# Layer 2's first projection by seven block products instead of eight

## The reference

```python
# attention: q, k, v [2, 8, 576, 64]; pooled (factor 4) plus a band of +-3 positions -> x [1152, 512]
h = x @ w_in                                  # layer 1: [1152, 512] @ [512, 2048]
g = np.where(h > 0.0, h, np.exp(np.minimum(h, 0.0)) - 1.0)
x = g @ w_out                                 # [2048, 512]
p = domain_probs / (domain_probs.sum(-1, keepdims=True) + 1e-09)
for e in range(4):                            # layer 2: 4 experts
    h = np.maximum(x @ w1[e], 0.0)            # [1152, 512] @ [512, 1024]: its first projection
    out += p[:, e:e + 1] * (h @ w2[e])        # [1024, 512]: the projection back
```

## Time and profile before

| | |
|---|---|
| median of 3 runs | 693.27 us (692.98 to 693.93) |
| span of the profiled execution | 692.0 us |
| TensorE busy | 678.2 us (98%) |
| VectorE, ScalarE, GpSimd busy | 300.9, 245.5, 217.4 us |
| layer 1, batch 1 (4 blocks) | from 189.83 to 292.55 us |
| layer 2 (8 halves) | from 292.55 us to the end |

### The profile page before, as it was taken

How to read it: one execution, slowest core, us unless ns; L and a number is a source line. 1 busy time by engine, 2 the same in 40 slices (tenths; PEclk the granted TensorE clock), 3 DMA queues, 4 the chain that set the end, 5 groups by cost and what they waited for, 6 DMA issues and landing times.

```text
span 692.0 us, 12297 instructions
## 1 busy us (share of the span) xinstructions
PE 678.2 (98%) x4558; PEld 625.7 (90%) x4564; DVE 300.9 (43%) x586; ACT 245.5 (35%) x665; POOL 217.4 (31%) x193
## 2 busy tenths in 40 slices
PE   7979999999999999999999999999999999999998
PEld 4659999999999999998898898998998998998986
DVE  3765666767695574542222222222222222223222
ACT  4664656556575474442031031130230220320310
POOL 5564444445437335222022022112211220220200
PEclk9998999999999999999999999999999999999999
DMA  9933161614212311311011011011011011000012
GB/s 207 191 79 96 62 143 54 166 38 143 62 62 62 118 65 61 122 62 62 0 62 62 0 61 61 0 61 61 0 61 61 0 61 61 26 35 0 0 43 93
DMA packets 51481, 46.01 MB, mean 66 GB/s; under 512 B 31616, under 2 KB 33920, under 8 KB 51456
## 3 DMA queue, kind: packets, MB, share of 16 engines
q1 hardware_dynamic: 51456, 45.67, 22.8%
HBM read 43.30 MB, written 2.36 MB: 66 GB/s over the span
## 4 chain that ended last, share of the span: by engine, by line
PE 89%; DVE 5%; ACT 2%; DMA 1%; issue 1%; POOL 1%; SPq 0%; DVEq 0%; ACTq 0%; POOLq 0%
PE psum L376 28%; PE psum L377 27%; PE psum L378 27%; PE psum L294 1%; DMA k_in<-in_k 1%; PE psum L368 1%; DVE h_lo L745 1%; PE psum L322 1%; ACT attn_p L527 1%; DVE elu_sum L739 1%; PE psum L281 1%; DVE x_lo L723 1%; DVE neg_max L688 1%; DVE elu_sum L733 1%; PE psum L313 1%
## 5 line engine op out<-in xcount | busy, mean ns | idle before, releaser
L376 PE MATMUL psum<-x_hi,wa_hi 128*128 128x384 f32 (+1 forms) x624 | 200.2, 321 | 0.0
L378 PE MATMUL psum<-x_hi,wa_lo 128*128 128x384 f32 (+1 forms) x624 | 199.2, 319 | 0.0
L377 PE MATMUL psum<-x_lo,wa_hi 128*128 128x384 f32 (+1 forms) x624 | 199.1, 319 | 0.0
L883 POOL TENSOR_TENSOR wb_lo<-wb_raw,wb_hi 128x512 fp32r<-128x512 f32 x64 | 85.4, 1339 | 239.7 <-ACT wb_hi L559 239.7
L599 ACT ACTIVATE h_hi<-psum 128x384 fp32r<-128x384 f32 x96 | 47.2, 492 | 291.3 <-PE psum L378 291.3
L376 PEld LDWEIGHTS psum<-x_hi,wa_hi 128*128 128x128 f32 x624 | 117.2, 188 | 0.9
L377 PEld LDWEIGHTS psum<-x_lo,wa_hi 128*128 128x128 f32 x624 | 117.2, 188 | 0.3
L378 PEld LDWEIGHTS psum<-x_hi,wa_lo 128*128 128x128 f32 x624 | 117.1, 188 | 0.0
L771 DVE SCALAR_TENSOR_TENSOR h_lo<-psum,h_hi 128x384 fp32r<-128x384 f32 x96 | 53.4, 558 | 143.7 <-ACT h_hi L599 143.7
L778 DVE SCALAR_TENSOR_TENSOR o_acc<-psum,gate_now,o_acc 128x512 f32<-128x512 f32 x72 | 54.1, 751 | 139.5 <-PE psum L378 139.5
L883 POOL TENSOR_TENSOR wa_lo<-wa_raw,wa_hi 128x512 fp32r<-128x512 f32 x60 | 76.0, 1300 | 121.5 <-ACT wa_hi L554 121.5
(11 more groups left out here) (94 smaller groups left out, 720.8 us busy)
## 6 DMA issues: line engine op xcount, KB each, us to landing
wa_raw<-in_moe_w_in SPq DMA_DIRECT2D x8, 1024.0 KB, 5.2
wb_raw<-in_moe_w_out SPq DMA_DIRECT2D x8, 1024.0 KB, 5.0
wa_raw<-in_moe_w SPq DMA_DIRECT2D x8, 1024.0 KB, 5.0
wb_raw<-in_moe_w SPq DMA_DIRECT2D x8, 1024.0 KB, 5.0
out<-o_acc SPq DMA_DIRECT2D x9, 256.0 KB, 2.0
q_in<-in_q SPq DMA_DIRECT2D x12, 144.0 KB, 4.0
k_in<-in_k SPq DMA_DIRECT2D x12, 144.0 KB, 4.1
v_in<-in_v SPq DMA_DIRECT2D x6, 288.0 KB
```

The source lines that it names most:

```text
L376: nc.tensor.matmul(bank_cols, w_hi(n), x_hi_(n), start=(n == 0), stop=False)
L377: nc.tensor.matmul(bank_cols, w_hi(n), x_lo_(n), start=False, stop=False)
L378: last = nc.tensor.matmul(bank_cols, w_lo(n), x_hi_(n), start=False, stop=(n == chunks - 1))
L883: nc.gpsimd.tensor_tensor(lo[:, c, :], raw[:, c, :], hi[:, c, :].bitcast(F32), ALU.subtract).then_inc(lo_ready, 1)
```

## The change

A half's first projection is done for each batch by itself (`step2`, two for a half). The operands are cut in 2 by 2 blocks: weights by 256 hidden columns and 256 channels, tokens by 288 tokens and 256 channels. In place of the 8 block products the result is put together from 7 (P1 to P7), with sums of weight blocks (S1, S2, S4 and, in place, one block of `wa_raw`), sums of token blocks (T1, T2, T4 and one block of `y_acc` in place) and sums of results. Each block product has two pairs p = 0, 1 (128 hidden columns each) of 6 matmuls with 288 columns.

The sums of weights (`add_w2`) are 4 GpSimd instructions for each half, queued behind the `wb` split, and there are 3 more operands to split (`s_hi`, `s_lo`). The sums of tokens (`add_y`) are 4 VectorE instructions for each batch, once, with 7 parts to split instead of 4, whose lo parts are moved to GpSimd (`split_y`). For batch 0 these stand inside block 4 of layer 1, before 4 blocks of work; for batch 1 they stand behind the last group of layer 1. The results' sums are VectorE instructions with one PSUM and one SBUF input; ScalarE copies P1 to SBUF. Three of the four hidden blocks then have their ReLU and lo part taken from SBUF sums. The projection back has 2 banks instead of 3. The buffers of the attention are given back to make room. `split_first2` puts the first split of layer 2's weights in groups 8 to 14 of block 7.

```diff
-DOWN2_BANKS = (0, 1, 2)
+DOWN2_BANKS = (7, 6)
+BANK_A, BANK_B, BANK_C = (0, 3), (1, 4), (2, 5)
...
-        elu_exp, elu_sum = sb("elu_exp", [128, 2, N1]), sb("elu_sum", [128, 2, N1])
+        sums2 = sb("sums2", [128, 3, PAIRS2, N2])
+        p1_sum, u2_sum, w_sum = sums2[:, 0], sums2[:, 1], sums2[:, 2]
...
+        s_raw = y_acc[:, 0:3, 0:2 * QF].rearrange("p s (k n) -> p s k n", k=2)
+
+        def t_raw(b, t):
+
+            return h_spare[:, T_RAW[t], b * SEQ:(b + 1) * SEQ].rearrange("p (k n) -> p k n", k=2)
...
+        def y_quad(b, kh, th):
+            return y_acc[:, 2 * kh:2 * kh + 2, b * SEQ + N2 * th:b * SEQ + N2 * (th + 1)]
...
+        def wa_quad(fh, kh):
+            return wa_raw[:, 2 * kh:2 * kh + 2, QF * fh:QF * (fh + 1)]
...
+            def step2(j, b):
+
+                v = 2 * j + b
...
+                pe.wait_ge(y_lo_ready, Y_PARTS * b + 2)
+                for p in range(PAIRS2):
+                    pe.wait_ge(h_lo_ready, UPS_LAYER1 + TILES_STEP * (v - 1) + p + 1)
+                    product2(bank(BANK_A, p), weights(0, 0, p), tokens(0, 0), True, False, p1_done)
+                pe.wait_ge(y_lo_ready, Y_PARTS * b + 3)
+                for p in range(PAIRS2):
+                    pe.wait_ge(moe_free, MOE_CREDIT + GROUPS_LAYER1)
+                    pe.wait_ge(c21_ready, PAIRS2 * v + p + 1)
+                    product2(bank(BANK_B, p), weight_sum(S2, p), token_sum(T2_), True, False, p6_done)
+                pe.wait_ge(y_lo_ready, Y_PARTS * b + 6)
+                for p in range(PAIRS2):
+                    pe.wait_ge(p1_copied, PAIRS2 * v + p + 1)
+                    product2(bank(BANK_A, p), weights(0, 1, p), tokens(1, 0), False, True, p2_done)
+                for p in range(PAIRS2):
+                    pe.wait_ge(c12_ready, PAIRS2 * v + p + 1)
+                    product2(bank(BANK_C, p), weight_sum(S1, p), token_sum(T1_), True, False, p5_done)
+                for p in range(PAIRS2):
+                    pe.wait_ge(u2_ready, PAIRS2 * v + p + 1)
+                    product2(bank(BANK_B, p), weights(1, 0, p), tokens(0, 1), False, False, p7_done)
+                for p in range(PAIRS2):
+                    pe.wait_ge(w_ready, PAIRS2 * v + p + 1)
+                    product2(bank(BANK_C, p), weight_sum(S4, p), tokens(1, 1), False, True, p3_done)
+                pe.wait_ge(y_lo_ready, Y_PARTS * b + 7)
+                for p in range(PAIRS2):
+                    pe.wait_ge(c22_ready, PAIRS2 * v + p + 1)
+                    product2(bank(BANK_B, p), weights(1, 1, p), token_sum(T4_), False, True, p4_done)
+
             def block2(e, half):
 
                 j = 2 * e + half
...
                 pe.wait_ge(wa_lo_ready, KC * (w + 1))
-                for g in range(UP2):
...
+            def split_first2(n):
+
+                act.wait_ge(wa_loaded, 16 * (2 * BLOCKS1 + 1))
+                act.wait_ge(group_done, groups_before1(2 * BLOCKS1 - 1) + UP1)
+                split_w2(0, n)
...
+                if n < KC:
+                    act.wait_ge(s_raw_ready, 4 * j + 3)
+                    nc.scalar.copy(wa_hi[:, n, :], wa_raw[:, n, :]).then_inc(wa_hi_ready, 1)
+                else:
+                    act.wait_ge(s_raw_ready, 4 * j + 4)
+                    nc.scalar.copy(s_hi[:, n - KC], s_raw[:, n - KC]).then_inc(s_hi_ready, 1)
...
+            def step2(j, b):
+
+                v = 2 * j + b
+                w = 2 * BLOCKS1 + j
...
+                def hidden_hi(fh, th, p, src):
+                    nc.scalar.activation(h_hi[:, 2 * fh + p, b * SEQ + N2 * th:b * SEQ + N2 * (th + 1)], src,
+                                         ACT.Relu).then_inc(h_hi_ready, 1)
+
+                for p in range(PAIRS2):
+                    act.wait_ge(p1_done, PAIRS2 * v + p + 1)
+                    act.wait_ge(h_lo_ready, UPS_LAYER1 + TILES_STEP * (v - 1) + 3 * PAIRS2 + p + 1)
+                    nc.scalar.copy(p1_sum[:, p], psum[:, BANK_A[p], 0:N2]).then_inc(p1_copied, 1)
+                if b == 0:
+                    split_wb(w, 0)
+                    split_wb(w, 1)
+                for p in range(PAIRS2):
+                    act.wait_ge(p2_done, PAIRS2 * v + p + 1)
+                    hidden_hi(0, 0, p, psum[:, BANK_A[p], 0:N2])
+                if b == 0:
+                    split_wb(w, 2)
+                for p in range(PAIRS2):
+                    act.wait_ge(c22_ready, PAIRS2 * v + p + 1)
+                    hidden_hi(1, 1, p, w_sum[:, p])
+                if b == 0:
+                    split_wb(w, 3)
+                for p in range(PAIRS2):
+                    act.wait_ge(c12_ready, UNIT_CREDIT + PAIRS2 * v + p + 1)
+                    hidden_hi(0, 1, p, u2_sum[:, p])
+                for p in range(PAIRS2):
+                    act.wait_ge(c21_ready, UNIT_CREDIT + PAIRS2 * v + p + 1)
+                    hidden_hi(1, 0, p, p1_sum[:, p])
...
                 if not last:
-                    for c in range(KC):
-                        split_wa(w + 1, c, GROUPS_LAYER1 + UP2 * (j + 1))
+                    act.wait_ge(wa_loaded, 16 * (2 * BLOCKS1 + j + 2))
+                    for n in range(KC + 3):
+                        split_w2(j + 1, n)
...
+                if n in (0, 1, 4, 5):
+                    c = n if n < 2 else n - 2
+                    act.wait_ge(t_raw_ready, 4 * b + 2)
+                    nc.scalar.copy(x_hi[:, c, b * SEQ:(b + 1) * SEQ],
+                                   y_acc[:, c, b * SEQ:(b + 1) * SEQ]).then_inc(y_hi_ready, 1)
+                else:
+                    t = {2: T2_, 3: T1_, 6: T4_}[n]
+                    act.wait_ge(t_raw_ready, 4 * b + {2: 3, 3: 1, 6: 4}[n])
+                    nc.scalar.copy(t_hi[:, t, :, b * N2:(b + 1) * N2], t_raw(b, t)).then_inc(y_hi_ready, 1)
...
-            act.wait_ge(moe_free, MOE_CREDIT + groups_before1(BLOCKS1))
-            for n in range(KC):
-                split_y(0, n)
+            after = {9 + n: [(split_y, 0, n)] for n in range(Y_PARTS)}
+            for g in range(GROUPS1):
+                group1(BLOCKS1, 1, g, after.get(g, ()))
+            with act.Fori(BLOCKS1 + 1, 2 * BLOCKS1 - 1) as w:
+                    group1(w, 1, g)
+            after = {UP1 + n: [(split_first2, n)] for n in range(KC + 3)}
+            for g in range(GROUPS1):
+                group1(2 * BLOCKS1 - 1, 1, g, after.get(g, ()), False)
+            for n in range(Y_PARTS):
                 split_y(1, n)
...
+                def add_p1(p, done, bank, dst, ready):
+                    dve.wait_ge(done, PAIRS2 * v + p + 1)
+                    dve.wait_ge(p1_copied, PAIRS2 * v + p + 1)
+                    nc.vector.tensor_tensor(dst[:, p], psum[:, bank[p], 0:N2], p1_sum[:, p], ALU.add).then_inc(ready, 1)
+
+                def hidden_lo(n, fh, th, p, src):
+                    at = (slice(None), 2 * fh + p, slice(b * SEQ + N2 * th, b * SEQ + N2 * (th + 1)))
+                    dve.wait_ge(h_hi_ready, UPS_LAYER1 + TILES_STEP * v + PAIRS2 * n + p + 1)
+                    nc.vector.scalar_tensor_tensor(h_lo[at], src, 0.0, h_hi[at].bitcast(F32),
+                                                   ALU.max, ALU.subtract).then_inc(h_lo_ready, 1)
+
+                for p in range(PAIRS2):
+                    add_p1(p, p6_done, BANK_B, u2_sum, u2_ready)
+                for p in range(PAIRS2):
+                    hidden_lo(0, 0, 0, p, psum[:, BANK_A[p], 0:N2])
+                for p in range(PAIRS2):
+                    add_p1(p, p5_done, BANK_C, w_sum, w_ready)
+                for p in range(PAIRS2):
+                    dve.wait_ge(p7_done, PAIRS2 * v + p + 1)
+                    dve.wait_ge(w_ready, PAIRS2 * v + p + 1)
+                    nc.vector.tensor_tensor(w_sum[:, p], psum[:, BANK_B[p], 0:N2], w_sum[:, p], ALU.add
+                                            ).then_inc(c22_ready, 1)
+                for p in range(PAIRS2):
+                    dve.wait_ge(p3_done, PAIRS2 * v + p + 1)
+                    dve.wait_ge(u2_ready, PAIRS2 * v + p + 1)
+                    nc.vector.tensor_tensor(u2_sum[:, p], psum[:, BANK_C[p], 0:N2], u2_sum[:, p], ALU.add
+                                            ).then_inc(c12_ready, 1)
+                    dve.wait_ge(y_lo_ready, Y_PARTS * (b + 1))
+                    hidden_lo(1, 1, 1, p, w_sum[:, p])
+                for p in range(PAIRS2):
+                    dve.wait_ge(w_ready, PAIRS2 * v + p + 1)
+                    add_p1(p, p4_done, BANK_B, p1_sum, c21_ready)
+                    hidden_lo(2, 0, 1, p, u2_sum[:, p])
+                for p in range(PAIRS2):
+                    hidden_lo(3, 1, 0, p, p1_sum[:, p])
+
...
+            def add_y(b, n):
+
+                if n == 0:
+                    dve.wait_ge(moe_free, MOE_CREDIT + groups_before1(BLOCKS1 * (b + 1)))
+                    nc.vector.tensor_tensor(t_raw(b, T1_), y_quad(b, 0, 1), y_quad(b, 0, 0), ALU.subtract
+                                            ).then_inc(t_raw_ready, 1)
+                elif n == 1:
```

(61 more changed lines are left out.)

145 lines of the change are left out of this document (90 added, 55 removed).

## The result

The changed kernel takes 713.34 us (median of 4 runs, 709.83 to 714.15); the kernel before, run beside it, 693.60 (692.98 to 695.10). The ratio is 1.028, 95% interval 1.025 to 1.031: slower by 20 us, twice the 10 of the forecast. It lies inside the stated range of 684 to 717, and just outside the 697 to 712 that the forecast gave itself. The profiled execution took 713.66 us, its span is 711.6.

What follows compares the result with a forecast made beforehand. TensorE, busy 98% of the span, was taken as the bound. The span, 692.0 - 20.7 - 0.3 + 18.2 + 3.9 + 3.6 + 2.5 + 3.2 = 702.4, plus 1.3 gave 703.7, forecast 703.5 us; range 684 to 717, its own 697 to 712.

Steps and rivals of the forecast that it cites:

- (b): Layer 1, blocks 4 and 5: late casts and GpSimd splits make TensorE wait for `wb_lo`, 3.6 us; bounds 2.5 and 5.3.
- The turns: Layer 2 halves: VectorE's two-SBUF-input instructions alternate with GpSimd's sums, 1.47 us a turn; stall 2.6 us in seven halves, 18.2 us.
- the timetable: Step-by-step times forecast for a half and the end of layer 1; in a half, lo parts end from 11.31 to 17.19 us.
- rival of cheap turns: VectorE instructions slip in beside GpSimd's without waiting out the hold; 679.4 us, or 685.5 if only halves are spared; chance 0.20.
- (a): Start of layer 2: ScalarE's seven batch 1 casts, queued before its first P1 copy, stall TensorE's P2 by 3.9 us.
- (c): Layer 1, block 7: the first half's `add_w2` falls among VectorE's pairs, stalling TensorE about 2.5 us; 2.0 to 3.6.
- (d): Around the end of layer 1: clock falls after the stalls of (a) and (b), 1.6 us each, 3.2 us; bounds 0 and 6.
- the clock falls in every half: Rival: the stall in each of 7 halves lowers the clock, 1.6 us each, 11 more: 715 us; chance 0.13.

Runs made afterwards that it cites:

- e1: Changed kernel with GpSimd's sums of weights held back until the half's last lo part is done; 686.6 us, ratio 0.989 to the kernel before.
- e8: Changed kernel with only the second two of the four weight sums of halves 2 to 8 held back; 698.07 us, ratio 1.007 to the kernel before.
- e2: Changed kernel with the weight sums of halves 2 to 8 replaced by one tiny sum and three write-only memsets; 685.65 us, ratio 0.987.
- e4: Changed kernel with batch 0's token casts behind block 4's weight casts and their lo parts behind the weight splits of blocks 5 and 6; 702.91 us.
- e7: e5 with the first half's weight sums also held back until block 7's last lo part, and TensorE's waits for split sums moved to P6 and P3; 680.49 us.
- e3: Changed kernel with batch 1's seven token casts moved on ScalarE from before the first P1 copy into the first half's first step; 708.8 us.
- e5: Changed kernel with the edits of e1, e3 and e4 together; 679.70 us, ratio 0.981 to the kernel before.

## Why the prediction was right, and short by ten

**The matmuls.** A first projection came down by 24.99 - 22.23 = 2.76 us, forecast 2.59: its 168 matmuls cost 132.3 ns each, not 133.3. The projection back stayed, at 24.50.

**The sum.** By span, 702.4 us was forecast and 711.6 measured. Of the 9.2 between them, 5.9 are the clock's falls from 190 us on, 3.2 the attention part and 1.1 the waits of layer 1; the matmuls gave 1.6 more than forecast, and 0.6 are left over. Two slips in the working change little: in (b), 41.5 - 38.4 is 3.1 and not 3.3, and the bounds of the terms add up to 696 and 713, not 697 and 712.

**The turns.** Right in mechanism and size: 2.6 us a half were forecast and 2.61 measured, with the lo parts' ends within 0.12 us of the timetable. Held back (e1), halved (e8) or made write-only (e2), the sums give back all, two thirds or all of it. The rival of cheap turns is out: L925 from SBUF took 766 ns on the mean beside the sums and 509 without. Two small errors cancel: GpSimd's sums took 1.37 to 1.50 us, longer than the 1.26 taken from the earlier trace rows, but a turn stayed at 1.46. In e1, away from such VectorE instructions, the sums took 1.28 to 1.30, so the rest is probably GpSimd's own wait for VectorE.

**The end of layer 1.** (a) 3.9 us forecast, 3.5 shown and 3.6 from start to start (310.81 - 303.99 less the 3.2 of P1 and P6). (b) 3.6 forecast, 3.45 shown, plus 0.72 for `wa_lo` of block 5, which the timetable had ready at 25.0 for a need at 25.6. (c) 2.5 forecast, 1.77 + 0.27 shown. The releasers are not the ones named: at block 5 the last was `h_lo` (VectorE, 236.04 us) where `wb_lo` was forecast (GpSimd's split ended at 235.7), and at block 7 it was VectorE's `y_acc`, late behind its lo parts, where `h_lo` was forecast. It is the same queue of turns in both: with the casts moved (e4) or the sums held back (e7) these waits were gone. L896 went from the 588 ns of the earlier trace rows to 834. Together layer 1's second batch was taken as 7.4 longer (with one fall, less the old wait) and was 8.2.

**The clock, the term that was mis-sized.** Step (d) took 3.2 us, two falls of 1.6, with 6 as its upper end, counted none in the halves, and gave the rival *the clock falls in every half* 0.13 with 11 us more. Measured: six falls from 190 us on in the first profile, 9.1 us, and nine in the second, one of them of double length, some 15 us. Three of the six halves 2 to 7 had one in the first profile and five in the second, and the first half had two in both. The size of a fall was right (1.5 us lost). What failed is the argument against it, that the stream is full on both sides of the wait, where the fall of the earlier trace rows stood among small matmuls, and with it a price for the waits alone that are longer than the 2.25 us of that gap: waits of 1.76 and 0.33 us with 0.8 us of matmuls between them had a fall behind them in 13 of 24 cases. One gap in the profile of before showed that a fall is possible; it could not show how short a wait may be. The rival was half true, and forecast plus half of its price (703.5 + 5.6 = 709) would have been the better number, though nothing on record then pointed at a half.

**Outside the forecast.** 3.2 us lie in the attention part, in code that the change does not touch. In e1 it ended at 189.5, in e2 at 186.9, and in the second profile of the changed kernel at 189.0. So it is no part of the change, and how much of it stands in the median is open; the first profiled run of the changed kernel had 17.1 us at the lower clock there, the kernel before 10.2.

## What to carry to other kernels

Before work is moved to GpSimd, list the VectorE instructions with two SBUF inputs that it will stand beside, and count one whole GpSimd instruction for each (in two profiles of twelve one of them waited out three or four); here four sums beside five such instructions cost 18 us and the falls behind them, and 13 us later in the same half they cost nothing. A stall of TensorE is to be priced with the clock that it may cost, 1.5 us more in half of the cases here for 2 us of rest. When one wait is removed, look at the engine that stands second at the same place: in e3, e5 and e7 a new wait took back a part of the gain or all of it.

## What the runs showed beside this

**Tiny VectorE instructions are held just as long.** The gate's instructions at the start of layer 2, by form, before:

```profile
L767 DVE COPY gate_now<-gate 128x9 f32 x4 | 0.7, 173 | 0.7 <-DVE gate L853 0.3
L849 DVE TENSOR_SCALAR gate_sum<-gate_sum 128x9 f32<-128x9 f32 x1 | 0.2, 174 | 0.0
```

and in the changed kernel, where GpSimd's lo parts of the tokens run beside them:

```profile
L1052 DVE TENSOR_SCALAR gate_sum<-gate_sum 128x9 f32<-128x9 f32 x1 | 1.2, 1157 | 0.0
L1054 DVE RECIPROCAL gate_sum<-gate_sum 128x9 f32<-128x9 f32 x1 | 0.2, 215 | 0.0
```

Nine elements took 1.16 us for 0.17. The forecast had counted only instructions with two SBUF inputs. TENSOR_SCALAR and COPY have one and were held as well (COPY 1.00 us in e3's rows above); RECIPROCAL was not: 0.22 us as before, beside a GpSimd instruction that was running. The Trainium skill, SBUF — State Buffer, section "Who interferes with whom", names copy and tensor_scalar among the instructions that can take the shared ports, when their operands meet its conditions, and these rows agree. A few such instructions in a row cost a microsecond each here, with nine elements: they are what e3 ran into.
